# Value product of an attention stage: V made the stationary operand, exponentials streamed in two column tiles, results turned back by transposes

## Chip, cores, metric

The kernel runs on one core of one Trainium2 chip. The metric is the device time in microseconds of one execution. The profile is of one such execution and gives each engine's instructions: TensorE (PE, with its weight loads as PEld), VectorE (DVE), ScalarE (ACT), GpSimd (POOL) and SyncE (SP).

## The reference

Three stages follow one another. The change touches the first alone, masked attention over 2 x 8 = 16 heads with 768 tokens and head width 64, all in float32:

```python
mask = q_bucket[:, :, :, None] == k_bucket[:, :, None, :]      # 6 hash bits of q and k
scores = np.where(mask, scale * q @ k.T, -1e9)
scores = scores - np.max(scores, axis=-1, keepdims=True)
attn = np.exp(scores)
attn = attn / (np.sum(attn, axis=-1, keepdims=True) + 1e-09)
return np.matmul(attn, v)
```

A query that matches no key gets equal weights, that is the mean of V. The heads side by side form x (2 x 768 x 512). Then comes a Fourier transform over tokens and features, added to x, with a wide MLP behind it, and last a gated MLP that mixes tokens.

## The kernel before

**Tiling.** The 768 tokens of a head are T = 6 tiles of 128, or two halves of HALF = 384. For head g and key tile kt, `scores` makes transposed scores (keys on partitions, queries along the row) in two PSUM banks, one per half: four products of 384 columns in the type fp32r. ScalarE's `exponentials` writes exp of them to `E[:, kt % 3]`, 128 keys by 768 queries in float32. `values(t, ahead, kt)` multiplies: for each query tile j, the stationary operand is the 128 x 128 block `E[:, kt % 3, tile(j)]`, the moving one `vn[:, s, kt, :]` of D1 = 65 columns (64 of V and a column of ones, whose product is the row sum). The result, queries on partitions, accumulates over kt in one PSUM bank per head, alternating between two banks. A float32 product is issued as two instructions, each with its own weight load; an fp32r product is one instruction. So a head has 36 products, 72 instructions, of this kind. One product more, `ones` x `vsum`, gives the sum of V.

**Order.** Each engine has a program of its own, and semaphores join them. The heads are a software pipeline, `one_time(it, u)`: in one head time TensorE does the six `scores` of head g, the six `scores_for_max` of head g+2, the transposes and hash products of head g+3, `max_rows` of head g+1, and the value products of head g with one key tile of delay, so that the last (kt = 5) falls in the next head time. `first_times()` is the written-out start for the heads up to 0, a loop runs over heads 1 to 12, and four more head times (u = 1 to 4) finish heads 13, 14 and 15. Each engine works strictly through its own list.

**End of a head.** After the sixth value product, VectorE's `head_output` (L1283 to L1291) takes reciprocals of the row sums and scales the PSUM bank into X; this stands in its list at kt == 1. GpSimd's `finish_head` (L464, L467) then makes `fill`, the mean of V for queries with no match, and adds it to X, which raises `x_done`. GpSimd also sums V (L476 to L481), issues two copies of operand halves and lowers a tile of W1 (L508), in a fixed order.

**Last heads.** In the head times u = 2 and u = 3 behind the loop, VectorE's list has, behind `head_output`, the folds of the Fourier stage (`fold_tokens` L1347, `fold_features` L1360, `fold_mirrored` L1367 to L1370). ScalarE has `fold_hi` between the exponentials of kt = 4 and kt = 5, and it waits for those folds; GpSimd has `fold_lo` (L524) at the end of its list for that head time. TensorE's next head can't start its scores until the exponentials of kt = 5 have emptied the score banks. After u = 4 TensorE goes on with `first_transform(0)`.

Of the kernel before, what the change touches and what calls it, by code (L numbers as in the profile page):

```python
# [21 lines left out]
D1 = D + 1  # L22
# [28 lines left out]
SLOTS = 4  # L51

# [6 lines left out]
def mixer_kernel(nc, q, k, v, proj, w_ch1, w_ch2, w_in, g_ln, w_sg, b_sg, w_out,  # L59
                 t1_hi, t1_lo, t2_hi, t2_lo, out):  # L60
    with ExitStack() as ctx:
# [32 lines left out]
        def run(at, *items):  # L94
            placed = []
            for name, shape, dt in items:
# [10 lines left out]
                   ("vn", [P, SLOTS, T, D1], F32), ("E", [P, 3, S], F32), ("mz", [P, 2, T, 2], F32R),  # L107
# [5 lines left out]
                   ("low_rows", [P, 2, HALF], F32), ("bit_off", [P, 2], F32))  # L113
# [7 lines left out]
        A = layout("a", t1 + attn + t2 + [("W1H", W1H_AT, [P, FT, KT, P], F32R),  # L121
# [49 lines left out]
        st_rdy, exp_done, vsum_step, pv_step = sems("st_rdy exp_done vsum_step pv_step")  # L171

        norm, pv_out, fill_done, x_done = sems("norm pv_out fill_done x_done")
# [74 lines left out]
        PV_FREE = 3  # L248
        OUT_FREE = 2
# [4 lines left out]
        ST_BANK, PV_BANK, SM_BANK, PREP_BANK = 0, 2, 4, 6  # L254

# [10 lines left out]
        MEAN_AT = 400  # L266
# [164 lines left out]
        def _(pool):  # L431
# [5 lines left out]
            pool.memset(A["vn"][:, :, :, D:D1], 1.0)  # L437
# [19 lines left out]
            def finish_head(t):  # L457

                g, s = t.head(-1), t.slot(-1)
                pool.wait_ge(pv_out, g + 1 + OUT_FREE)  # L460
# [3 lines left out]
                pool.tensor_tensor(A["fill"][:, :, :], z, mean, ALU.mult).then_inc(fill_done, 1)  # L464
                pool.wait_ge(fill_done, g + 1)
                xh = head_out(t.it, t.u - 1)
                pool.tensor_tensor(xh, xh, A["fill"][:, :, :], ALU.add).then_inc(x_done, 1)  # L467

# [13 lines left out]

            def one_time(it, u):
                t = Time(it, u)
                if not t.looped and t.it < 0:
# [7 lines left out]
                else:  # L493
# [6 lines left out]
                    if t.has(1):  # L500
                        sum_values(t, 1)
                if t.has(-1):
                    finish_head(t)
                if t.has(0):

                    f = t.head(0)
                    pool.wait_ge(w1_hi, f + 1)
                    pool.tensor_tensor(M1["W1L"][:, f, :, :], A["W1R"][:, f, :, :], rd(A["W1H"][:, f, :, :]),  # L508
                                       ALU.subtract).then_inc(w1_lo, 1)
# [104 lines left out]
        def _(pe):  # L614
# [85 lines left out]
            def values(t, ahead, kt, tiles=range(T)):  # L700
                g, s, bank = t.head(ahead), t.slot(ahead), PV_BANK + t.slot(ahead, 2)
                if kt == 0 and 0 in tiles:
                    pe.wait_ge(v_in[s], 32 * t.turn(ahead) + 32)
                    pe.wait_ge(vsum_step, 3 * g + 3)
                    pe.wait_ge(pv_out, g - 1 + OUT_FREE)

                    mm(PS[:, bank, MEAN_AT:MEAN_AT + D], ones[:, :], A["vsum"][:, s, :], True, True)
                pe.wait_ge(exp_done, 2 * T * g + 2 * kt + 2 + EXP_FREE)
                for j in tiles:
                    last = mm(PS[:, bank, j * D1:(j + 1) * D1], A["E"][:, kt % 3, tile(j)], A["vn"][:, s, kt, :],  # L710
                              False, kt == T - 1, skip_group_check=True)
                if T - 1 in tiles:
                    last.then_inc(pv_step, 1)
# [6 lines left out]
            def first_times():  # L720
# [3 lines left out]

                a, b = range(TH), range(TH, T)
# [34 lines left out]
                values(fill0, 0, 0, a)  # L760
                scores_for_max(fill1, 3)
                values(fill0, 0, 0, b)
# [3 lines left out]
                values(fill0, 0, 1, a)  # L766
                both(hash_bits, fill1, 1)
                scores_for_max(fill1, 5)
                values(fill0, 0, 1, b)
# [842 lines left out]
```

## Time and profile before

| | us |
|---|---|
| median of 3 runs | 773.26 (770.96 to 773.28) |
| profiled execution, its time | 773.6 |
| its span, first to last instruction | 771.8 |
| TensorE matmul busy | 756.7 (98%) |
| TensorE weight load busy | 695.7 (90%) |
| VectorE, ScalarE, GpSimd busy | 404.3, 277.4, 201.9 |

About 1.8 us of the profiled time lie outside the span. A matmul's record starts when its columns begin to stream; its end is modelled and overlaps the next, so the pace of a run of matmuls is read from starts: (length of a row less length of its last record) divided by (count less one). A row of the timeline may merge several instructions (xN).

### The profile page before, as it was taken

How to read it: one execution, taken by the hardware profiler on the slowest of the kernel's cores; microseconds unless marked ns; L12 is line 12 of the kernel's file. 1: busy time of each engine (PE TensorE's matmuls, PEld its weight loads, DVE VectorE, ACT ScalarE, POOL GpSimd, SP SyncE). 2: the span in 40 equal slices, each digit the busy share in tenths (PEclk: the TensorE clock that was granted, in tenths of full speed). 3: DMA queues.
4: the chain of work that ended last, by engine and by line, in shares of the span. 5: the costliest groups of instructions: out<-in, count | busy, mean ns of one | idle time of the engine just before them, and what ended most of it. 6: DMA issues, size and time to landing. Idle time of an engine off the chain costs nothing.

```text
span 771.8 us, 12918 instructions
## 1 busy us (share of the span) xinstructions
PE 756.7 (98%) x4614; PEld 695.7 (90%) x4614; DVE 404.3 (52%) x746; ACT 277.4 (36%) x585; POOL 201.9 (26%) x258
## 2 busy tenths in 40 slices
PE   8999999999999999899999999999999999999998
PEld 7889999999999989899999999989999887888886
DVE  7887777677776658731132214123113487337733
ACT  4456666666665543411121112111113453015401
POOL 4133223332233563395000000000013146003300
PEclk9999999999999999999999999999999999999999
DMA  5233333223311500260000000000031000010001
GB/s 126 57 86 82 86 74 79 70 65 91 82 44 45 192 2 1 82 247 0 1 0 0 0 0 1 0 0 0 1 123 55 15 1 1 27 56 0 0 14 68
DMA packets 55569, 36.14 MB, mean 47 GB/s; under 512 B 40048, under 2 KB 48240, under 8 KB 55024
## 3 DMA queue, kind: packets, MB, share of 16 engines
q1 hardware_dynamic: 52720, 26.76, 12.2%
q0 software_dynamic: 2816, 8.94, 4.3%
q8 instruction: 21, 0.34, 0.2%
q14 instruction: 12, 0.10, 0.0%
HBM read 27.03 MB, written 3.15 MB: 39 GB/s over the span
## 4 chain that ended last, share of the span: by engine, by line
PE 90%; DVE 7%; issue 1%; ACT 1%; POOL 1%; DVEq 0%; POOLq 0%; ACTq 0%
PE PS L616 86%; DVE mneg L1264 2%; PE PS L631 1%; DVE ops L1244 1%; DVE Z L1360 1%; PE PS L937 1%; PE PS L979 1%; PE PS L883 1%; PE PS L905 1%; DVE fold L1347 0%; DVE Y L1367 0%; DVE ops L1234 0%; DVE Y L1368 0%; DVE ops L1231 0%; POOL vr L574 0%
## 5 line engine op out<-in xcount | busy, mean ns | idle before, releaser
L616 PEld LDWEIGHTS PS<-vn,E 128*128 128x128 f32 x1152 | 140.9, 192 | 1.6 <-ACT E L1037 1.4
L616 PE MATMUL PS<-vn,E 128*128 128x65 f32 x1152 | 140.6, 271 | 1.3 <-ACT E L1037 1.3
L1450 DVE SCALAR_TENSOR_TENSOR hL<-PS,hH 128x384 fp32r<-128x384 f32 x64 | 35.7, 558 | 201.5 <-ACT hH L1160 201.5
L616 PE MATMUL PS<-ops 98*128 98x384 f32 (+1 forms) x576 | 128.3, 354 | 2.0 <-DVE mneg L1264 1.5
L1264 DVE TENSOR_REDUCE mneg<-PS 128x1 f32<-128x768 f32 x96 | 91.8, 958 | 52.2 <-PE PS L616 51.0
L1160 ACT ACTIVATE hH<-PS 128x384 fp32r<-128x384 f32 x64 | 31.5, 492 | 227.2 <-PE PS L616 227.2
L1037 ACT ACTIVATE E<-PS 128x384 f32<-128x384 f32 x192 | 83.7, 487 | 77.5 <-PE PS L616 76.1
L616 PEld LDWEIGHTS PS<-ops 98*128 98x128 f32 (+1 forms) x576 | 96.5, 190 | 4.0 <-DVE mneg L1264 2.0
L616 PE MATMUL PS<-unTH,W1L 128*128 128x384 f32 x256 | 86.4, 337 | 0.0
L616 PE MATMUL PS<-unTH,W1H 128*128 128x384 f32 x256 | 86.2, 337 | 0.0
L616 PE MATMUL PS<-unTL,W1H 128*128 128x384 f32 x256 | 85.9, 336 | 0.0
L616 PE MATMUL PS<-W2H,hL 128*128 128x512 f32 x192 | 75.9, 395 | 0.0
L616 PE MATMUL PS<-W2L,hH 128*128 128x512 f32 x192 | 75.7, 395 | 0.0
L616 PE MATMUL PS<-W2H,hH 128*128 128x512 f32 x192 | 75.6, 394 | 0.0
L1023 ACT ACTIVATE ops<-PS 64x384 fp32r<-64x384 f32 (+1 forms) x96 | 44.8, 481 | 35.9 <-PE PS L616 20.8
L616 PEld LDWEIGHTS PS<-unTH,W1H 128*128 128x128 f32 x256 | 48.1, 188 | 2.6
L616 PEld LDWEIGHTS PS<-unTL,W1H 128*128 128x128 f32 x256 | 48.0, 188 | 2.5
L616 PEld LDWEIGHTS PS<-unTH,W1L 128*128 128x128 f32 x256 | 48.0, 188 | 0.0
L616 PEld LDWEIGHTS PS<-W2H,hL 128*128 128x128 f32 x192 | 36.0, 188 | 7.7
L616 PEld LDWEIGHTS PS<-W2L,hH 128*128 128x128 f32 x192 | 36.1, 188 | 6.0
L616 PEld LDWEIGHTS PS<-W2H,hH 128*128 128x128 f32 x192 | 36.1, 188 | 5.7
L565 POOL TENSOR_TENSOR WinL<-WinR,WinH 128x512 fp32r<-128x512 f32 x8 | 10.3, 1290 | 115.3 <-ACT WinH L1023 115.3
(178 smaller groups left out, 1298.7 us busy)
## 6 DMA issues: line engine op xcount, KB each, us to landing
ops<-ops POOLq DMA_DIRECT2D x28, 192.0 KB, 3.0
W1R<-in_moe_w_ch_dram SPq DMA_DIRECT2D x16, 256.0 KB, 2.8
W2R<-in_moe_w_ch_dram SPq DMA_DIRECT2D x4, 1024.0 KB, 6.9
qk<-in_k_dram SPq DMA_DIRECT2D x32, 96.0 KB, 2.8
qk<-in_q_dram SPq DMA_DIRECT2D x32, 96.0 KB, 2.8
vn<-in_v_dram SPq DMA_DIRECT2D x32, 96.0 KB, 2.8
out_dram<-X SPq DMA_DIRECT2D x12, 256.0 KB, 2.1
WsgR<-in_moe_w_sg_dram SPq DMA_DIRECT2D x1, 2304.0 KB, 7.9
```

The costliest lines, as they stand in the source:

```text
L565: pool.tensor_tensor(M2["WinL"][:, c // 2, cols], R1["WinR"][:, c // 2, cols], rd(M2["WinH"][:, c // 2, cols]), ALU.subtract).then_inc(win ...
L616: return pe.matmul(dst, lhs, rhs, start=start, stop=stop, **kw)
L631: last = pe.transpose(PS[:, bank, tile(c)], A["qk"][:, t.slot(3, 2), a * TH + c, :], ident[:, :])
L883: last = pe.transpose(PS[:, un_bank(n, kt), tile(c)], M1["un"][:, c, tile(kt)], ident[:, :])
L905: last = pe.transpose(PS[:, 5 + n % 3, tile(c)], R2["WsgR"][:, r, at:at + TH * (P - 1) + 1:TH], ident[:, :])
L937: last = pe.transpose(PS[:, 6 + j % 2, tile(kt)], M2["xs"][:, j % 2, tile(kt)], ident[:, :])
L979: last = pe.transpose(PS[:, 6 + j % 2, tile(kt)], M2["gated"][:, j % 2, tile(kt)], ident[:, :])
L1023: return act.activation(dst, src, ACT.Copy, scale=scale)
L1037: act.activation(A["E"][:, kt % 3, half(a)], PS[:, ST_BANK + a, 0:HALF], ACT.Exp, scale=EXP_SCALE).then_inc(exp_done, 1)
L1160: act.activation(M1["hH"][:, f % 2, :], PS[:, f % 2, 0:HALF], ACT.Relu).then_inc(hhi_done, 1)
L1264: dve.tensor_reduce(A["mneg"][:, s, j:j + 1], PS[:, max_banks(t, j):max_banks(t, j) + 2, 0:HALF], AX.XY, ALU.max, negate=True).then_inc(ma ...
L1450: dve.scalar_tensor_tensor(M1["hL"][:, f % 2, :], PS[:, f % 2, 0:HALF], 0.0, rd(M1["hH"][:, f % 2, :]), ALU.max, ALU.subtract).then_inc(hl ...
```

## The change

`values` now takes a part (0, 1, 2) of two key tiles each. V's tile (128 x 64) is stationary, and the exponentials stream past it, one half of 384 queries to the output partitions 0 to 63, the other to 64 to 127, in `PV_BANK`. The column of ones in `vn` goes. GpSimd adds exponentials over key tiles (`sum_exponentials`, four additions of 128 x 768 per head into `esumA` and `esumB`), and parts 1 and 2 multiply these with ones into `SUM_BANK`. `E` has four buffers in place of three. ScalarE copies both banks to `outT` (`raw_output`); TensorE turns them back (`turn_back`, at kt == 3 of the next head time): three transposes and three products of two columns for the row sums. VectorE's part is split into `value_mean` at kt == 1 and `head_output` at kt == 3. On GpSimd the fill and the lowering of W1 stand apart from `finish_head`, W1's one head later. The value parts of the first head and of each head time move to new places in TensorE's list.

```diff
+            def fill_head(t):
+                g, s = t.head(-1), t.slot(-1)
+                pool.wait_ge(mean_done, g + 1 + MEAN_FREE)
...
+            def sum_exponentials(t, ahead, step):
+                g = t.head(ahead)
+                dst = A["esumA"] if step < 2 else A["esumB"]
+                kt = (1, 2, 4, 5)[step]
+                pool.wait_ge(exp_done, 2 * T * g + 2 * kt + 2 + EXP_FREE)
+                if step % 2 == 0:
+                    if t.looped or g:
+                        pool.wait_ge(pv_step, PV_PARTS * (g - 1) + (2 if step == 0 else 3))
+                    first = A["E"][:, e_slot(t, ahead, kt - 1), :]
+                else:
+                    pool.wait_ge(esum_step, SUM_STEPS * g + step)
+                    first = dst[:, :]
+                pool.tensor_tensor(dst[:, :], first, A["E"][:, e_slot(t, ahead, kt), :], ALU.add).then_inc(esum_step, 1)
...
             def one_time(it, u):
                 t = Time(it, u)
+                if t.has(-1):
+                    sum_exponentials(t, -1, 3)
...
+                if t.has(0):
+                    sum_exponentials(t, 0, 0)
                 if t.has(-1):
+                    fill_head(t)
+                if t.has(0):
+                    sum_exponentials(t, 0, 1)
+                if t.has(-1):
+                    w1_lower(t)
                     finish_head(t)
                 if t.has(0):
...
+                    sum_exponentials(t, 0, 2)
...
+            def values(t, ahead, part):
+                g, s = t.head(ahead), t.slot(ahead)
+                if part == 0:
                     pe.wait_ge(v_in[s], 32 * t.turn(ahead) + 32)
+                    pe.wait_ge(mean_done, g + MEAN_FREE)
                     pe.wait_ge(vsum_step, 3 * g + 3)
+                    mm(PS[:, PV_BANK, MEAN_AT:MEAN_AT + D], ones[:, :], A["vsum"][:, s, :], True, True)
+                pe.wait_ge(exp_done, 2 * T * g + 4 * part + 4 + EXP_FREE)
+                for kt in (2 * part, 2 * part + 1):
+                    for a in range(2):
+                        last = mm(PS[a * D:(a + 1) * D, PV_BANK, 0:HALF], A["vn"][:, s, kt, :],
+                                  A["E"][:, e_slot(t, ahead, kt), half(a)], kt == 0, kt == T - 1)
+                if part:
+                    if part == 1:
+                        pe.wait_ge(pv_out, g + OUT_FREE)
+                    pe.wait_ge(esum_step, SUM_STEPS * g + 2 * part)
+                    sums = A["esumA"] if part == 1 else A["esumB"]
+                    for a in range(2):
+                        last = mm(PS[a * D:(a + 1) * D, SUM_BANK, 0:HALF], ones[:, 0:D], sums[:, half(a)],
+                                  part == 1, part == 2)
+                last.then_inc(pv_step, 1)
+
+            def turn_back(t):
+                g, s = t.head(-1), t.slot(-1)
+                pe.wait_ge(raw_done, g + 1)
+                for c in range(TH):
+                    pe.transpose(PS[:, SUM_BANK, tile(c)], A["outT"][:, 0, tile(c)], ident[:, :])
+                for c in range(TH):
+                    last = mm(PS[:, SUM_BANK, DEN_AT + 2 * c:DEN_AT + 2 * c + 2], A["outT"][:, 1, tile(c)],
+                              ident[:, 0:D + 1:D], True, True)
+                last.then_inc(ot_rdy, 1)
...
                 for kt in range(T):
                     if t.has(0):
                         scores(t, kt)
+                    if kt == 3 and t.has(-1):
+                        turn_back(t)
                     if t.has(2):
                         scores_for_max(t, kt)
...
-                    if kt == 0 and t.has(-1):
-                        values(t, -1, T - 1)
-                    if kt >= 1 and t.has(0):
-                        values(t, 0, kt - 1)
-                    if kt == 1 and t.has(1):
+                    if kt == 1 and t.has(-1):
+                        values(t, -1, 2)
+                    if kt == 2 and t.has(1):
                         max_rows(t, 0)
                         max_rows(t, 1)
+                    if kt in (3, 5) and t.has(0):
+                        values(t, 0, kt // 2 - 1)
...
+            def raw_output(t):
+                g = t.head(-1)
+                act.wait_ge(pv_step, PV_PARTS * g + PV_PARTS)
+                act.wait_ge(ot_rdy, g + TURN_FREE)
+                copy(A["outT"][:, :, :], PS[:, PV_BANK:PV_BANK + 2, 0:HALF]).then_inc(raw_done, 1)
...
                     if kt == 1 and t.has(-1):
-                        head_output(t)
+                        value_mean(t)
                     if kt in (3, 4) and t.has(3):
                         bit_rows(t, kt - 3)
+                    if kt == 3 and t.has(-1):
+                        head_output(t)
```

## Rows read from the trace of the kernel before

**Rows 1.** The page, busy shares and the granted clock in 40 slices.
```profile
PE 756.7 (98%) x4614; PEld 695.7 (90%) x4614; DVE 404.3 (52%) x746; ACT 277.4 (36%) x585; POOL 201.9 (26%) x258
...
PEclk9999999999999999999999999999999999999999
```

**Rows 2.** Stages: length, then busy us of PE, PEld, DVE, ACT, POOL; clock; DMA.
```profile
0.00:42.00 42.00, 37.33 (x248) 33.02 (x248) 33.56 (x62) 19.17 (x38) 12.55 (x31) 1.00 0.42 93
...
197.68:214.06 16.38, 16.38 (x127) 16.32 (x127) 12.41 (x26) 10.37 (x25) 5.38 (x9) 1.00 0.32 76
...
250.00:300.00 50.00, 47.69 (x363) 46.93 (x362) 30.03 (x46) 20.78 (x47) 28.17 (x22) 0.93 0.21 75
```

**Rows 3.** Groups by form on TensorE, 100 to 198 us: count, busy, mean ns.
```profile
L616 PE MATMUL PS<-vn,E 128*128 128x65 f32 x434 | 52.9, 271 | 0.0
```

**Rows 4.** Timeline of TensorE over one head time: start, length, count.
```profile
197.68 0.33 PE L616 MATMUL PS<-vsum,ones 128*128 128x64 f32 x2
197.85 1.50 PE L616 MATMUL PS<-vn,E 128*128 128x65 f32 x12
199.16 0.55 PE L616 MATMUL PS<-ident_r,mz 128*2 128x128 f32 x6
...
213.18 1.04 PE L616 MATMUL PS<-ops 128*128 128x384 f32 x5
214.06 0.33 PE L616 MATMUL PS<-vsum,ones 128*128 128x64 f32 x2
```

**Rows 5.** Timeline of TensorE in narrow windows, for the starts of successive float32 matmuls.
```profile
203.42 0.22 PE L616 MATMUL PS<-vn,E 128*128 128x65 f32 x1
...
203.47 0.39 PE L616 MATMUL PS<-vn,E 128*128 128x65 f32 x2
...
8.09 0.38 PE L616 MATMUL PS<-ident 128*128 128x128 f32 x2
...
8.20 0.50 PE L616 MATMUL PS<-ident 128*128 128x128 f32 x3
```

**Rows 6.** GpSimd: two groups by form, 50 to 250 us, then one of the timeline.
```profile
L467 POOL TENSOR_TENSOR X<-X,fill 128x384 f32 x12 | 12.0, 1002 | 3.8 <-POOL fill L464 3.8
L464 POOL TENSOR_TENSOR fill<-nomatch,vmean 128x384 f32<-128x384 f32 x13 | 10.8, 830 | 15.4 <-DVE X L1291 15.4
...
261.05 2.28 POOL L464 TENSOR_TENSOR fill<-nomatch,vmean 128x384 f32<-128x384 f32 x1 [3.76 <-DVE X L1291]
```

**Rows 7.** Timeline of the head time u = 2 (head 14), all engines.
```profile
257.51 0.95 PE L616 MATMUL PS<-ops 98*128 98x384 f32 x4
258.15 0.87 ACT L1037 ACTIVATE E<-PS 128x384 f32<-128x384 f32 x2 [1.52 <-PE PS L616]
259.79 0.17 DVE L1283 TENSOR_SCALAR den<-PS 128x6 f32<-128x6 f32 x1 [1.96 <-PE PS L616]
260.89 1.75 DVE L1347 TENSOR_TENSOR fold<-X 128x1536 f32<-128x1536 f32 x1
268.69 0.15 DVE L1370 COPY Y<-Z 128x3 f32<-128x3 f32 x1
268.88 1.48 ACT L1023 ACTIVATE yHL<-Y 128x1536 fp32r<-128x1536 f32 x1 [1.11 <-DVE Y L1370]
270.37 0.85 ACT L1037 ACTIVATE E<-PS 128x384 f32<-128x384 f32 x2
270.98 0.94 PE L616 MATMUL PS<-ops 98*128 98x384 f32 x4 [0.43 <-ACT E L1037]
```

**Rows 8.** Timeline behind head 15, and the stage 286 to 293 us.
```profile
284.17 3.43 POOL L524 TENSOR_TENSOR yHL<-Y,yHL 128x1536 fp32r<-128x1536 f32 x1 [3.46 <-ACT z0H L1023]
284.91 1.63 PE L616 MATMUL PS<-vn,E 128*128 128x65 f32 x12 [1.25 <-ACT E L1037]
286.30 0.51 PE L616 MATMUL PS<-T1H,yHL 128*128 128x194 f32 x1
...
286.00:293.00 7.00, 7.00 (x38) 6.77 (x37) 3.48 (x8) 0.59 (x2) 6.31 (x5) 0.52 0.00 0
```

**Rows 9.** The chain that ended last, 0 to 60 us, by line.
```profile
by line: PE PS L616 48.3%; DVE mneg L1264 20.9%; DVE ops L1244 10.6%; issue 4.9%; DVE ops L1234 4.7%; DVE ops L1231 4.0%; PE PS L631 3.3%; ACT ops L1023 0.8%; POOL ident L435 0.5%; DVE pjL L1297 0.4%; POOL ident L432 0.3%; POOL pj L433 0.2%
```

More of the change, by code:

```diff
@@ L21 @@
 FT = F // P
-D1 = D + 1
 LN_EPS = 1e-6
@@ L51 @@
 SLOTS = 4
+E_SLOTS = 4
 def token_tiles(ap):
@@ L247, in mixer_kernel @@
         EXP_FREE = 2
-        PV_FREE = 3
-        OUT_FREE = 2
+        MEAN_FREE = 1
+        TURN_FREE = 1
+        OUT_FREE = 1
         MAX_FREE = 1
@@ L254, in mixer_kernel, with e_slot @@
         ST_BANK, PV_BANK, SM_BANK, PREP_BANK = 0, 2, 4, 6
+        SUM_BANK = PV_BANK + 1
+        PV_PARTS, SUM_STEPS = 3, 4
+        def e_slot(t, ahead, kt):
+            return (T * t.slot(ahead, 2) + kt) % E_SLOTS
         def max_banks(t, j):
@@ L467, in finish_head, with w1_lower @@
                 pool.tensor_tensor(xh, xh, A["fill"][:, :, :], ALU.add).then_inc(x_done, 1)
+            def w1_lower(t):
+                f = t.head(-1)
+                pool.wait_ge(w1_hi, f + 1)
+                pool.tensor_tensor(M1["W1L"][:, f, :, :], A["W1R"][:, f, :, :], rd(A["W1H"][:, f, :, :]),
+                                   ALU.subtract).then_inc(w1_lo, 1)
             def sum_values(t, step):
@@ L704, in values @@
                     pe.wait_ge(vsum_step, 3 * g + 3)
[L705 to L711, printed above, removed]
@@ L1034, in exponentials @@
                     act.wait_ge(st_rdy, 2 * T * g + 2 * kt + a + 1)
-                    if a == 0:
-                        act.wait_ge(pv_step, T * g + kt - 2 + PV_FREE)
-                    act.activation(A["E"][:, kt % 3, half(a)], PS[:, ST_BANK + a, 0:HALF], ACT.Exp,
+                    if a == 0 and kt % 2 == 0 and (t.looped or g or kt == T - 2):
+                        act.wait_ge(pv_step, PV_PARTS * g + kt // 2 - 1)
+                    if a == 0 and kt in (1, T - 2) and (t.looped or g or kt == T - 2):
+                        act.wait_ge(esum_step, SUM_STEPS * (g - 1) + 3 if kt == 1 else SUM_STEPS * g + 1)
+                    act.activation(A["E"][:, e_slot(t, 0, kt), half(a)], PS[:, ST_BANK + a, 0:HALF], ACT.Exp,
                                    scale=EXP_SCALE).then_inc(exp_done, 1)
@@ L1057, in rows_of_maximum @@
                          PS[0:2, row_bank(t, a), 0:HALF]).then_inc(m_done, 1)
+            def raw_output(t):
+                g = t.head(-1)
+                act.wait_ge(pv_step, PV_PARTS * g + PV_PARTS)
+                act.wait_ge(ot_rdy, g + TURN_FREE)
+                copy(A["outT"][:, :, :], PS[:, PV_BANK:PV_BANK + 2, 0:HALF]).then_inc(raw_done, 1)
             def w1_upper(t):
@@ L1090, in one_time @@
                         upper_halves(t)
-                    if kt == 1 and t.has(1):
+                    if kt == 1 and t.has(-1):
+                        raw_output(t)
+                    if kt == 2 and t.has(1):
                         rows_of_maximum(t)
@@ L1277, in split_maximum, with value_mean @@
                                   ALU.subtract).then_inc(split_done, 1)
[L1279 to L1285 removed]
+            def value_mean(t):
+                g = t.head(-1)
+                dve.wait_ge(raw_done, g + 1)
+                dve.wait_ge(x_done, g - 1 + X_FREE)
+                dve.tensor_scalar(A["vmean"][:, t.slot(-1, 2), :], PS[:, PV_BANK, MEAN_AT:MEAN_AT + D], 1.0 / S, None,
+                                  ALU.mult).then_inc(mean_done, 1)
+            def head_output(t):
+                g, s = t.head(-1), t.slot(-1)
+                dve.wait_ge(ot_rdy, g + 1 + TURN_FREE)
+                den = PS[:, SUM_BANK, DEN_AT:DEN_AT + T].rearrange("p (c a) -> p a c", a=2)
+                dve.tensor_scalar(A["den"][:, :].rearrange("p (a c) -> p a c", a=2), den, DEN_EPS, None, ALU.add).then_inc(norm, 1)
                 dve.wait_ge(norm, 3 * g + 1)
```

55 lines of the change are left out of this document (18 added, 37 removed).

## The prediction

> **What bounds the kernel now.** First the page: TensorE has matmuls in flight for 98% of the span, at the full 2.4 GHz (granted clock 9 tenths or more in every slice) [rows 1]. Then the busy table by stage, to see whether that holds where the change acts. One steady head time, from one product of `vsum` to the next, takes 214.06 - 197.68 = 16.38 us [rows 4]. In it TensorE is never idle, VectorE is busy 12.4, ScalarE 10.4, GpSimd 5.4 us [rows 2]. So in the loop TensorE's own list sets the pace. In the start the chain of waits is shared with VectorE (20.9% in `mneg` alone) [rows 9], and in the last heads TensorE has pauses (47.69 busy in 50 us) and the clock's mean drops to 0.93 [rows 2]. These three stretches are costed apart. Then the timeline row by row.
>
> **What is removed.** Twelve value matmuls start at an even pace of (1.45 to 1.50 less 0.27) / 11 = 0.112 us [rows 3, 4]. The two shortest steps of the trace show why: behind 384 columns, whose time hides a weight load, the second matmul of 65 columns starts 0.05 to 0.06 us after the first [rows 5]; the steady 0.112 is the load of 128 float32 columns. So 72 x 0.112 = 8.05 us per head go.
>
> **What is added on TensorE.** No float32 matmul of 384 columns exists in the trace. Those of 65 columns take 0.055 us, those of 128 take 8.20 - 8.09 = 0.11 [rows 5], both 0.86 ns per column. The fp32r ones of 384 columns start every (1.04 - 0.34) / 4 = 0.175 us, 0.46 ns per column, with 0.015 above a plain 0.16 [rows 4]. A float32 stream thus costs two cycles a column, and 384 columns 0.32 + 0.015 = 0.335 us, call it one unit. Bounds: 0.175 if the doubling vanished, 0.34.
>
> A head has 6 x 2 value products and 2 x 2 sum products, 32 instructions. If nothing runs side by side that is 32 units, 10.7 us. If the two column tiles run fully side by side it is 16 units, 5.36 us. I take the tiles as independent but matmuls as starting in the order of the list. Then of each half its two instructions follow each other in the same tile, and only the second of one half overlaps the first of the other. A part of two key tiles takes 5 units, not 4; with its sums 7, not 6. Per head 5 + 7 + 7 = 19 units, 6.37 us. No row shows column tiles at work, which is the largest doubt here.
>
> By the Trainium skill (TensorE: Matmul & The Clock Gate, measured speedup of packing), three column tiles gave 2.38 times the rate; as an estimate two would give 1.59, so 32 / 1.59 = 20 units, 6.7 us. No row here shows it, and my sum doesn't use it.
>
> `turn_back` is three transposes and six matmuls, all with 128 stationary columns: 9 x 0.11 = 1.0 us. The mean's product stays.
>
> TensorE now changes between full width and half width six times a head. The nearest row is the group with two stationary columns: twelve value matmuls from 197.85 should end at 199.19 and the next group starts at 199.16 [rows 4], so a change of width there cost nothing that shows. The other bound is a full emptying of the array, about 271 - 112 = 159 ns, the part of a record that overlaps the next [rows 3]. I take 0.02 each, 0.1 a head, as the nearest row is near zero. The Trainium skill (TensorEngine Tiling (Array Packing), key properties) says a change of tiling mode drains the engine. By that the six would cost up to 1.0 us a head; it is a rival below.
>
> Steady head: -8.05 + 6.37 + 1.0 + 0.1 = -0.6 us. Thirteen head times run so (heads 1 to 13): -7.8 us.
>
> **What hides the rest.** Four additions of 128 x 768 per head on GpSimd: 384 elements take 1.00 us and 1536 take 3.43 [rows 6, 8], so 768 about 1.8, and 7.2 a head. GpSimd then has 12.6 of 15.8 us, and in order: it waits for operand halves until some 3.8 us into the head time (transposes to 1.7, then four ScalarE copies of 0.49), does its small work to 6.2, the first sum to 8.0, fill, second sum to 10.7, W1, finish to 13, third sum to 14.8, and the fourth ends 0.9 us into the next. TensorE asks for the last at 4.4 and for the second at 14.5, so both are hidden by over 3 us. Uncovered, each would put its whole 1.8 us on TensorE's path. ScalarE's copy of 768 columns, some 0.82 us (half of 0.87 plus a little, 0.49, for 384; 1.48 for 1536) [rows 7], brings it to 11.2. Its result is asked for two key tiles later. VectorE's work stays at 12.4. A load of V waits for the end of a head three back, which stays far in the past, so SP's queue is not moved.
>
> **The start.** Twelve units replace 60 matmuls (4.0 against 6.7 us), but much of this stretch follows VectorE's chain [rows 9], and the exponentials of kt = 4 now wait for GpSimd's first sum, which stands behind the operand copies; `max_rows` copies and hash bits queue behind them on ScalarE. I count +0.5 us, bounds -2 and +3.
>
> **The last heads: the cost.** In u = 2 `head_output` starts 259.79 - 257.51 = 2.3 us after the head time does. Behind it in VectorE's list are the folds, until 268.8; ScalarE's `fold_hi` waits for them, 268.88 to 270.4; behind it are the last exponentials, and behind these the next head's scores at 270.98 [rows 7]. So these head times (13.5 us) are set by this chain and not by TensorE, and what delays `head_output` delays everything. It now follows `turn_back`. Built up from the start: scores 0.7, scores of kt = 1 held by the exponentials to 1.65, part 2 to 4.0, ScalarE's copy to 4.9, exponentials (0.87 a pair) to 5.8, scores of kt = 3 to 6.15, `turn_back` to 7.15. That is 4.9 us later. In u = 3 the same 4.9, and more: GpSimd's fourth sum now stands behind `fold_lo`, 3.4 us long after `fold_hi`, so TensorE gets it at 5.0 and not 3.3, +1.7. After head 15, the value product took 286.30 - 284.91 = 1.4 us before the transform began [rows 8]. Now: `fold_lo` to 2.9 us, fourth sum to 4.7, its product 0.7, copy 0.9, turning 1.0, so 7.5, +6.1. Together 4.9 + 6.6 + 6.1 = 17.6. A pause of 1.25 us was followed by 7 us at clock 0.52, that is at 1.2 GHz [rows 8]; pauses of 4 to 5 us before u = 3 and in u = 4 put part 2 and the turning at half rate, about +2.4 beyond what was lost before. Tail: +20 us. Bounds: +14, if the clock holds and the sums find room; +27, if GpSimd's additions beside VectorE's folds stretch both (a fill there took 2.28 us in place of 0.83 [rows 6]).
>
> **Sum.** 773.6 - 7.8 + 0.5 + 20 = 786.3, against the profiled 773.6; the runs' median of 773.26 is 0.3 lower, so 786.
>
> **Rivals.**
> - *Each width change empties the array.* Six times 0.16 in place of 0.02, +0.85 a head, thirteen times: +11, 797. For it: the page named above. Against it: the row at 199.16.
> - *The tiles do not overlap.* 32 units: -8.05 + 10.7 + 1.1 = +3.8 a head, +49; the tail some 24, the start +3: about 850. For it: no row of column tiles. Against it: nothing in the rows but that weight loads of the next matmul run beside the present one.
> - *The tiles overlap without the stagger* (the other side). 16 units of 0.325, 5.2 us: -1.8 a head, -23, less the tail's 19: about 769, faster. It decides once a head saves more than 20 / 13 = 1.5 us. For it: the two tiles use separate banks of rows in PSUM. Against it: a float32 product's two instructions share a tile and start in order. A stream of one cycle a column would give about 743; rows 5 speak against it.
> - *The tail's loss just cancels the loop's gain*, for instance tail 14 and -1 a head: about 774.
>
> **How the numbers follow.** Chances: my forecast 0.50, emptying 0.14, no overlap 0.15, no stagger or a fast stream 0.15, cancelled 0.06. The forecast's own range is 776 to 798. The range 766 to 806 leaves out the case without overlap and 0.05 at the edges. A measurement of this kernel can tell 0.3%, 2.3 us, from no change: faster 0.15, same 0.06, slower 0.79.
>
> **What would show it.** Right: pairs of value matmuls with 0.33 us between two starts and two that start nearly together; a head time of 15.7 to 15.9 us with TensorE busy throughout; no TensorE wait for `esum` in the loop; in u = 2 and u = 3 head times of 18 us or more, with TensorE waiting for E while ScalarE waits for Y; a dip of the clock there; the first transform 7 us or more after the last exponentials. Wrong: starts evenly 0.33 apart, head times near 20 us; or head times below 15 us; or GpSimd's additions well over 2 us each, which would make GpSimd the bound at 2.5 us.

## The result, and the profile after

The changed kernel takes 839.57 us (median, 839.06 to 842.45) against 773.26: ratio 1.087, 95% interval 1.084 to 1.091. The forecast was 786 with a range of 766 to 806, so the time lies 34 us above the range. The profiled execution is the longest of four (842.45 us) and has a span of 840.6 us (771.8 before).

The page of the kernel after: busy time, the granted clock in 40 slices, the chain that ended last by engine, and one group of VectorE (busy us, mean ns, idle time ahead).

```profile
PE 777.5 (92%) x4118; PEld 626.1 (74%) x4118; DVE 443.5 (53%) x746; ACT 289.2 (34%) x601; POOL 317.5 (38%) x321
...
PEclk9989999999999898699999999999999999999999
...
PE 71%; DVE 11%; issue 10%; POOL 5%; ACT 1%; DVEq 1%; POOLq 0%; ACTq 0%
...
L1322 DVE TENSOR_SCALAR ops<-ops,bit_off 12x768 fp32r<-12x768 f32 x24 | 45.0, 1913 | 0.0
```

Three things differ from [rows 1]. TensorE is no longer busy nearly throughout (92% for 98%). VectorE's busy time rose by 39 us with the same 746 instructions, so some of them became longer. One group alone explains 31 of these: the subtraction of `bit_off`, 24 times 1.91 us; in the kernel before, the same 24 instructions took 0.60 each (shortest, median, longest in ns; from and to in us):

```profile
L1258 DVE TENSOR_SCALAR ops<-ops,bit_off x24: 600/604/607, 60.8 to 241.2; 12x768 fp32r<-12x768 f32 x24
```

What TensorE waited for, in the kernel after and, last row, in the kernel before (us in total, times, longest):

```profile
PE PS L659 <- DVE mneg L1328: 32.7, 28, 2.2
PE PS L659 <- ACT E L1092: 12.9, 6, 6.0
...
PE PS L659 <- POOL esumB L518: 1.8, 1, 1.8
...
PE PS L616 <- DVE mneg L1264: 1.5, 5, 0.5
```

The wait for `mneg`, the maximum, was 1.5 us in five waits before; it now comes about twice a head and makes 32.7 us. The second row is mainly the two long waits of the last heads. The busy table, one head time of the kernel after (from one product of `vsum` to the next; columns as in [rows 2]), and the end of the last head:

```profile
200.16:219.96 19.80, 17.62 (x97) 12.09 (x97) 15.16 (x26) 11.07 (x24) 13.02 (x13) 0.91 0.26 63
...
343.00:361.00 18.00, 11.51 (x46) 8.20 (x47) 3.14 (x11) 3.73 (x7) 11.17 (x7) 0.53 0.01 1
```

A head time that was 16.38 us [rows 2] is 19.80. TensorE has 2.2 us of idle time in it and a mean clock of 0.91. The timeline of the kernel after shows how that comes about (start, length; in brackets the idle time before it and what ended it):

```profile
210.05 0.62 PE L659 MATMUL PS<-ops 76*128 76x384 f32 x2 [2.07 <-DVE mneg L1328]
...
211.10 2.27 PE L659 MATMUL PS<-ops 98*128 98x384 f32 x6
...
215.95 1.33 PE L659 MATMUL PS<-ops 98*128 98x384 f32 x6
...
220.22 1.51 PE L659 MATMUL PS<-E,vn 128*64 128x384 f32 x8
...
224.81 1.82 POOL L518 TENSOR_TENSOR esumB<-E 128x768 f32<-128x768 f32 x1
...
225.28 3.86 DVE L1322 TENSOR_SCALAR ops<-ops,bit_off 12x768 fp32r<-12x768 f32 x2
...
226.71 2.02 POOL L518 TENSOR_TENSOR esumB<-esumB,E 128x768 f32<-128x768 f32 x1
226.97 0.98 PE L659 MATMUL PS<-ops 98*128 98x384 f32 x4
...
229.17 0.96 DVE L1328 TENSOR_REDUCE mneg<-PS 128x1 f32<-128x768 f32 x1
...
230.18 0.62 PE L659 MATMUL PS<-ops 76*128 76x384 f32 x2 [2.23 <-DVE mneg L1328]
```

Read it from GpSimd. Its third addition starts at 224.81. VectorE's first subtraction starts at 225.28, inside it, and ends only after it (at 227.04 by its own record, against 226.63). The second meets the fourth addition and ends at 229.14, after 228.73. So `mneg` of the next head, next in VectorE's list, starts at 229.17, and TensorE, which needs the bank that this maximum reads, stands idle for 2.23 us until 230.18. One head earlier it is the same (2.07 us until 210.05), and what follows shows there: the clock is granted at half rate, 1.2 GHz, and six products take 2.27 us at 211.10 that take 1.33 at full clock at 215.95. Such a half-rate stretch of 3.4 us stands in most head times.

By the first exponentials of each head (before, then after; us), the 68.8 us between the two spans fall like this:

| stretch | before | after | more | forecast |
|---|---|---|---|---|
| start, to head 1 | 46.5 | 53.1 | +6.6 | +0.5 |
| heads 1 to 13, 12 head times | 196.7 | 233.0 | +36.3 | -7.2 |
| u = 1 | 14.95 | 20.6 | +5.7 | -0.6 |
| u = 2, u = 3 and up to the transform | 28.2 | 49.0 | +20.8 | +20 |
| the rest | | | -0.6 | 0 |

The tail came as forecast. The loop has the wrong sign, and the start is outside its bounds.

### The profile page after: what moved, and what is told of

Same layout as the page of the kernel before. It is cut to its first block, busy times and chain, and to the rows that moved or that the text cites. A ratio compares the mean times of both kernels' runs of the same rounds, so it can differ in the third digit from the quotient of the medians.

```text
span 840.6 us, 12169 instructions
## 1 busy us (share of the span) xinstructions
PE 777.5 (92%) x4118; PEld 626.1 (74%) x4118; DVE 443.5 (53%) x746; ACT 289.2 (34%) x601; POOL 317.5 (38%) x321
## 4 chain that ended last, share of the span: by engine, by line
PE 71%; DVE 11%; issue 10%; POOL 5%; ACT 1%; DVEq 1%; POOLq 0%; ACTq 0%
PE PS L659 67%; DVE mneg L1328 3%; DVE ops L1322 3%; POOL esumB L518 2%; DVE ops L1315 2%; PE PS L674 1%; POOL esumA L518 1%; POOL X L482 1%; PE PS L990 1%; PE PS L1032 1%; PE PS L936 1%; PE PS L769 1%; PE PS L958 0%; DVE ops L1308 0%; DVE wgt L1358 0%
## 5 line engine op out<-in xcount | busy, mean ns | idle before, releaser
L659 PE MATMUL PS<-ops 98*128 98x384 f32 (+1 forms) x576 | 149.8, 386 | 40.3 <-DVE mneg L1328 32.7
L659 PEld LDWEIGHTS PS<-ops 98*128 98x128 f32 (+1 forms) x576 | 103.4, 206 | 82.7 <-DVE mneg L1328 41.2
L659 PE MATMUL PS<-E,vn 128*64 128x384 f32 x384 | 81.1, 548 | 6.0 <-ACT E L1092 6.0
L659 PEld LDWEIGHTS PS<-E,vn 128*64 128x64 f32 x384 | 25.7, 150 | 38.5 <-issue 27.4
L1322 DVE TENSOR_SCALAR ops<-ops,bit_off 12x768 fp32r<-12x768 f32 x24 | 45.0, 1913 | 0.0
```

The lines of the kernel that those rows point to most:

```text
L659: return pe.matmul(dst, lhs, rhs, start=start, stop=stop, **kw)
L1322: dve.tensor_scalar(rows, rd(rows), A["bit_off"][BITROW:KMAX, key:key + 1], None, ALU.subtract).then_inc(mask_done, 1)
```

## The experiments

The median of the kernel before beside these runs was 772.2 to 773.5 us. Kernels 1, 3, 4, 6 and 7 were executed once, the others 4 to 10 times. The theory throughout is that GpSimd's additions hold up VectorE's subtractions; against it stood the later place of `head_output`, a list of GpSimd that had become too long, and TensorE's own new work. "Head time" is the distance of two heads' first exponentials in the loop; the one from head 1 to head 2, which differs from the others, is left out. In 2, 3, 4, 8 and 9 the time came out 0.2 to 3.9 us above the range of the theory that held, in 5 and 7 it came out 0.1 and 7.4 us below.

**1. Short sums.** GpSimd's four additions per head cover 64 of 768 columns.

```diff
...
-                pool.tensor_tensor(dst[:, :], first, A["E"][:, e_slot(t, ahead, kt), :], ALU.add).then_inc(esum_step, 1)
+                pool.tensor_tensor(dst[:, 0:D], first, A["E"][:, e_slot(t, ahead, kt), 0:D], ALU.add).then_inc(esum_step, 1)
...
```

> The changed kernel, with GpSimd's four additions per head cut from 768 columns to 64 (the row sums are then wrong). Theory A: the loop is slow because GpSimd's long additions keep VectorE's SBUF-to-SBUF subtraction (L1322, 1.91 us instead of 0.60) from running, VectorE's chain reaches over the next head's first maximum, TensorE pauses and drops to 1.2 GHz. Then the subtraction is back at 0.60 us, a head time falls from 19.5 to 15.3-16.2 us, and the time to 775-790 us. Theory B: VectorE's chain is too long because head_output moved between the hash bits and the maxima of kt 3 and 4; then the head time stays above 18.5 us and the time above 820 us.

784.74 us. The head time falls to 15.9 to 16.1 (one of 16.4), the subtraction to 0.64 us, the time to head 1 from 53.1 to 48.9. The row sums are wrong in this kernel. Fifty-five of the 66 us hang on how long GpSimd's additions last. Which neighbour they hurt, this run doesn't tell.

**2. Sums behind the bits.** The full additions stay; the third only waits until VectorE has subtracted.

```diff
                 if t.has(0):
+                    if t.has(3) and (t.looped or t.it >= 0):
+                        pool.wait_ge(mask_done, 2 * t.head(3) + 2)
                     sum_exponentials(t, 0, 2)
```

> The changed kernel with one wait more: GpSimd starts the third addition of a head only when VectorE's subtraction of the hash rows is done; all work stays. Theory A (the two must not run together): subtraction 0.60 us, head time 15.5-16.5 us, 785-800 us in all. Theory B (position of head_output): no change, 835-845 us. Theory C (GpSimd's list is simply too long, 13 us a head): later additions make it worse, over 845 us.

800.24 us, ratio to before 1.036 (1.034 to 1.038). With the same work and one wait more, 39 us come back. The trace of this kernel, VectorE's subtraction by tile (ns: shortest, median, longest) and the timeline of the same place:

```profile
L1324 DVE TENSOR_SCALAR ops<-ops,bit_off x24: 600/604/606, 66.6 to 247.5; 12x768 fp32r<-12x768 f32 x24
```

```profile
198.03 1.13 DVE L1324 TENSOR_SCALAR ops<-ops,bit_off 12x768 fp32r<-12x768 f32 x2
199.19 0.96 DVE L1330 TENSOR_REDUCE mneg<-PS 128x1 f32<-128x768 f32 x1
199.41 1.83 POOL L518 TENSOR_TENSOR esumB<-E 128x768 f32<-128x768 f32 x1 [1.79 <-DVE ops L1324]
200.19 1.08 DVE L1336 CAST mz<-mneg 128x6 fp32r<-128x6 f32 x1
```

The maximum at 199.19 reads PSUM and takes its usual 0.96 us while the addition runs. The CAST of six columns at 200.19 has both operands in SBUF; it takes 1.08 us, not 0.17, and ends with the addition (201.27 against 201.24). So instructions of VectorE that work within SBUF can stand still during an instruction of GpSimd; those that read PSUM don't. Not all within SBUF do. In the kernel after, beside GpSimd's lowering of W1:

```profile
181.48 1.29 POOL L488 TENSOR_TENSOR W1L<-W1R,W1H  x1
...
182.00 0.19 DVE L1356 RECIPROCAL rec<-den 128x6 f32<-128x6 f32 x1
182.23 0.57 DVE L1358 TENSOR_TENSOR wgt<-rec,match 128x6 f32<-128x6 f32 x1
```

The reciprocal has both operands in SBUF and takes its usual 0.19 us; the product of two SBUF tiles behind it takes 0.57 for 0.17. Held in these traces are the subtraction, the CAST and instructions with two inputs in SBUF. In kernel 2 the head time is 16.3 to 16.8 and the clock no longer falls in the loop.

**3. The subtractions on ScalarE**, behind its last exponentials; the additions stay where the change put them.

```diff
...
+                    act.activation(rows, rd(rows), ACT.Identity,
+                                   bias=A["neg_off"][BITROW:KMAX, key:key + 1]).then_inc(mask_done, 1)
...
```

> The changed kernel with the two subtractions of L1322 moved from VectorE to the end of ScalarE's list for a head time; the additions stay where they were. Theory A: it is these two instructions that are kept from running, so the head time falls to 15.8-16.5 us though GpSimd is as busy as before, and the time to 788-800 us. If the additions disturb VectorE in another way too (reductions or products out of PSUM), the head time stays above 17.5 us and the time above 812 us.

800.55 us, head time 16.3 to 16.5 (one of 18.8). One head of this kernel:

```profile
214.41 1.83 POOL L518 TENSOR_TENSOR esumB<-E 128x768 f32<-128x768 f32 x1
214.70 1.75 ACT L1125 ACTIVATE ops<-ops,neg_off 12x768 fp32r<-12x768 f32 x2
216.31 1.88 POOL L518 TENSOR_TENSOR esumB<-esumB,E 128x768 f32<-128x768 f32 x1
```

ScalarE works within SBUF beside the same additions, at 0.9 us each and without being held. Two quite different edits that only part the subtractions from the additions give the same 800. Neither edit shortens GpSimd's list or moves `head_output`, so a list of GpSimd that had become too long, or the later place of `head_output`, is not what holds up the loop.

**4. Idle products in the pause.** Eight products of 112 columns into unused columns of `SUM_BANK`, ahead of the maximum's scores.

```diff
+                    if kt == 0 and t.has(2) and (t.looped or t.it >= 0):
+                        for _ in range(8):
+                            mm(PS[:, SUM_BANK, 400:512], ident[:, :], ident[:, 0:112], False, True, skip_group_check=True)
```

> The changed kernel with eight idle float32 products (16 matmuls of 112 columns, 1.8 us) on TensorE at the place of its pause, before the first scores for the maximum of each head. If the drops of the clock behind the pauses are a cost of their own, the stretches at 1.2 GHz vanish from the loop and the slow heads (19.9 us) come down to about 18.5: 820-828 us. If the clock is only a by-product, the time stays at 836-842 us.

831.23 us. The subtraction is still at 1.92 us. The half-rate stretches are gone from the loop and the head time is 18.6 to 18.9. So the clock is worth some 8 us of the loss, and the pause itself, with VectorE's chain behind it, the rest of what the loop lost.

**5. The same addition in the kernel before.** Three additions of 128 x 768 on data that nobody uses, behind the exponentials of kt = 4.

```diff
...
+                    pool.wait_ge(exp_done, 2 * T * g + 10 + EXP_FREE)
+                    for n in range(3):
+                        pool.tensor_tensor(A["dumB"][:, :], A["dumA"][:, :], A["dumA"][:, :], ALU.add).then_inc(dum, 1)
...
```

> The kernel before, with three idle GpSimd additions of 128x768 in a row behind the exponentials of kt 4 in each head time of the loop; nobody waits for them. Theory A: the subtraction (L1258 there, 0.60 us) grows to 1.2-2.2 us, VectorE's last maximum of a head comes 1-2 us later, head time 16.36 to 17-18 us, 782-795 us in all. Theory B: the subtraction stays at 0.60 us and the time at 772-775 us.

781.88 us, ratio 1.011 (1.010 to 1.013). Head time 17.17 for 16.36. By tile, and in the timeline:

```profile
L1270 DVE TENSOR_SCALAR ops<-ops,bit_off x24: 600/1208/1818, 60.4 to 249.9; 12x768 fp32r<-12x768 f32 x24
```

```profile
213.57 5.15 POOL L520 TENSOR_TENSOR dumB<-dumA 128x768 f32<-128x768 f32 x3
215.05 2.34 DVE L1270 TENSOR_SCALAR ops<-ops,bit_off 12x768 fp32r<-12x768 f32 x2
```

Nothing of the change but the additions is in this kernel, on other tensors, and the same instruction is held. It is the additions as such, not `E`, PSUM or the new order.

**6. Half by half.** On top of 2, the four instructions of one half before the four of the other.

```diff
-                for kt in (2 * part, 2 * part + 1):
-                    for a in range(2):
+                for a in range(2):
+                    for kt in (2 * part, 2 * part + 1):
```

> The kernel with the sums behind the hash bits (800 us), with the value products of a part in another order: both key tiles of the first half of the queries, then both of the second. If matmuls only run side by side with the next in the list, as the prediction had it, a part's eight matmuls take 7 x 0.32 us in place of 4, head time +2.9 us, and the time 835-845 us. If what runs side by side are the two matmuls of one float32 product, nothing changes: 797-803 us.

800.0 us: no change. In the after kernel value matmuls start in pairs 6 to 7 ns apart, 0.32 us from pair to pair. Here they start in pairs 13 ns apart, again 0.31 to 0.32 us from pair to pair, and a part still takes four steps. I first read this as the two instructions of one float32 product running side by side, whatever the tile. Run 7 tests that.

**7. One tile.** On top of 2, both halves go to partitions 0 to 63, in one accumulation; the upper 64 partitions of the output stay stale, and the attention output is the sum of two halves.

```diff
-                        last = mm(PS[a * D:(a + 1) * D, PV_BANK, 0:HALF], A["vn"][:, s, kt, :],
-                                  A["E"][:, e_slot(t, ahead, kt), half(a)], kt == 0, kt == T - 1)
+                        last = mm(PS[0:D, PV_BANK, 0:HALF], A["vn"][:, s, kt, :],
+                                  A["E"][:, e_slot(t, ahead, kt), half(a)], kt + a == 0, kt + a == T)
...
```

> Edit: the kernel in which GpSimd's third addition stands behind VectorE's bit subtractions (800.24 us, head time 16.4), and in it both halves of the value products and of the sums go to the output partitions 0 to 63; so the two halves are summed into one result, the upper 64 partitions of the output are stale, and attention is wrong for every query. The number and shape of the matmuls stay. Theory (the two instructions of one float32 product with 64 stationary columns run beside each other, whichever column tile they write): starts stay in pairs some 10 ns apart, 0.32 us from pair to pair, time 799 to 802. Rival (the overlap needs both column tiles, as the prediction assumed): the matmuls start evenly 0.32 apart, 32 units a head instead of 16, some 5 us more per head, 870 us or more.

862.61 us, and the rival's picture: even starts 0.32 us apart, 32 units a head, head time 20.9. Part 2 of this kernel, then of kernel 6:

```profile
203.87 2.79 PE L661 MATMUL PS<-E,vn 128*64 128x384 f32 x8
206.50 1.45 PE L661 MATMUL PS<-esumB,ones 128*64 128x384 f32 x4
```

```profile
201.59 1.52 PE L661 MATMUL PS<-E,vn 128*64 128x384 f32 x8
202.93 0.82 PE L661 MATMUL PS<-esumB,ones 128*64 128x384 f32 x4
```

So my reading of run 6 falls, and the column tiles do work side by side: exactly twofold here. Together the two runs say more. When the second tile's first matmul is two instructions behind in the list, it starts 6 to 7 ns after the first tile's; when it is four behind, 13 ns. That fits some 3.3 ns for each instruction passed, and a matmul that doesn't wait until those ahead of it in the list for the other tile have started. The records don't name the tile, so this order is inferred, not seen: from the two spacings, and from four steps for eight matmuls of which the list has four of one tile ahead of four of the other. The sums of kernel 6, whose order wasn't changed, start 13 ns apart as well, so the distance may simply be carried on from the products ahead of them.

**8. The tail.** On top of 2, VectorE folds tokens and features at the start of the head times u = 2 and u = 3 and mirrors behind `value_mean`; `fold_lo(1)` stands behind the last addition.

```diff
...
+                if not t.looped and tail_pass(t) is not None:
+                    n = tail_pass(t)
+                    dve.wait_ge(x_done, H + X_FREE)
+                    fold_tokens(n)
+                    fold_features(n)
                 for kt in range(T):
...
+                    if kt == 1 and not t.looped and tail_pass(t) is not None:
+                        fold_mirrored(tail_pass(t))
...
-                if not t.looped and tail_pass(t) is not None:
-                    fold_lo(tail_pass(t))
+                if not t.looped and tail_pass(t) == 0:
+                    fold_lo(0)
...
```

> The kernel with the sums behind the hash bits (800 us), with the last heads mended: in head times u = 2 and 3 VectorE folds before it waits for the turned-back outputs, and GpSimd's second fold_lo stands behind the last head's last addition. Theory: of the 27 us by which the stretch from head 14 to the first transform is longer than before (48.6 against 28.2 us from the first exponentials of head 14), most is head_output's new place ahead of the folds. Then u = 2 and u = 3 take 13-15 us each and the time is 783-789 us. If TensorE's or ScalarE's own work is the bound there, over 795 us.

790.12 us, ratio 1.021 (1.020 to 1.023): 10 us back. The edit moves two things. u = 2, where only the folds moved, takes 15.0 us in place of 19.6. From the last exponentials' end to the first transform, where `fold_lo` moved, it is 4.7 us in place of 9.0. u = 3 up to there is 1.5 us longer.

**9. And the start.** On top of 8, in the written-out start GpSimd makes the first two additions ahead of its wait for operand halves.

```diff
...
+                    if t.has(0):
+                        sum_exponentials(t, 0, 0)
+                        sum_exponentials(t, 0, 1)
                     if t.head(3) >= 2:
                         pool.wait_ge(hi_done, 4 * t.head(3) + 4)
                         move_halves(t)
...
```

> The last one, with the start mended too: for head 0 GpSimd makes its first two additions before it waits for the operand halves of head 3. The first exponentials of head 1 then come at 47-48 us in place of 51-53 us (before: 46.5), and the time is 779-786 us, still a little above the kernel before, because a head time of 16.4 us saves nothing on one of 16.36. If GpSimd was not what delayed the start: as the tail alone.

789.89 us, ratio 1.021 (1.020 to 1.023). Head 1 starts at 48.8 in place of 51.3. Not all of the 2.5 us are the edit's: kernel 8 runs 6.9 us at half clock before head 1, kernel 9 only 3.4. Kernel 6, whose GpSimd list for the start is the one of 8, also has 3.4 us at half clock there, and head 1 at 50.0. So at the same clock the queue position of that addition held the start by 1.2 us (one execution each); the whole time doesn't gain by it beyond what can be told. What is left stands in u = 3 of this kernel:

```profile
280.15 3.41 POOL L574 TENSOR_TENSOR yHL<-Y,yHL 128x1536 fp32r<-128x1536 f32 x1
...
283.68 1.79 POOL L518 TENSOR_TENSOR esumB<-esumB,E 128x768 f32<-128x768 f32 x1
283.80 4.98 DVE L1441 TENSOR_TENSOR Z<-fold 128x768 f32<-128x768 f32 x2 [6.26 <-POOL z0L L576]
285.44 2.53 POOL L518 TENSOR_TENSOR esumA<-E 128x768 f32<-128x768 f32 x1
...
285.53 1.55 PE L666 MATMUL PS<-esumB,ones 128*64 128x384 f32 x4 [5.16 <-POOL esumB L518]
```

`fold_lo` stands ahead of the fourth addition and TensorE waits 5.2 us for it. Beside VectorE's folds both sides stretch: the addition to 2.53 us for 1.8, and two folds of features to 4.98 us, where in kernel 11 below, with nothing beside them, two take 1.83.

**10. All mended, sums nearly free.** Kernel 9 with the short additions of 1 (row sums wrong for most queries).

> Edit: all mended orders together (third addition behind the bit subtractions, first head's additions before the operand copies, folds first in the last heads; 789.89 us so far), and GpSimd's additions cut to 64 of 768 columns; the other 704 columns of the sums hold constants, so the row sums are wrong for most queries. It shows what the rest of the change is worth when the additions cost nothing. Theory (what keeps a head time at 16.3 us is still the additions beside VectorE's work, and the additions behind fold_lo in the tail): head time 15.1 to 15.9, tail 4 us shorter, 770 to 778 us: no better than before, as the turning back and the longer chain at the tail eat TensorE's gain. Rival (the order of the list, not the additions, holds the head time at 16.3): head time 16.2 or more, 785 or more.

771.42 us, ratio 0.999 (0.998 to 1.001). One head time of this kernel:

```profile
185.80:201.70 15.90, 15.61 (x96) 10.93 (x95) 12.39 (x26) 10.91 (x24) 6.52 (x12) 1.00 0.32 78
```

VectorE is back at 12.4 us and TensorE's own list is 15.6, 0.8 below the 16.38 of [rows 2]. That is what the new value product is worth at best. Both kernels reach the first transform at 286.3 us: the start takes 1.1 us more, the twelve head times 3.2 less (16.1 each on average, with waits, for 16.4), and the stretch from there 2.2 more, of which 1.9 lie behind head 15's first exponentials (16.6 us to the transform for 14.7).

**11. The kernel before with folds first.** The VectorE part of 8 in the kernel before, with the mirrors behind `head_output`.

> Edit: the kernel before, with the folds of tokens and features at the head of VectorE's list in the head times u = 2 and u = 3 and the mirrored fold behind head_output. It tells whether the tail of the kernel before also follows the chain head_output, folds, fold_hi, exponentials. Theory: ScalarE's fold_hi waits 1.1 us less, the next scores start 1 to 3 us earlier in each of the two head times: 768 to 771 us. Rival (GpSimd's fold_lo or TensorE's own list sets the tail; VectorE's folds meet GpSimd's work and head_output comes later): 773 or more.

768.63 us, ratio 0.995 (0.994 to 0.997): the one version that beats both kernels. Its trace:

```profile
257.76 1.75 DVE L1348 TENSOR_TENSOR fold<-X 128x1536 f32<-128x1536 f32 x1
...
259.54 1.83 DVE L1361 TENSOR_TENSOR Z<-fold 128x768 f32<-128x768 f32 x2
...
267.67 1.49 ACT L1023 ACTIVATE yHL<-Y 128x1536 fp32r<-128x1536 f32 x1
...
284.20 0.34 PE L616 MATMUL PS<-T1H,yHL 128*128 128x194 f32 x1
```

ScalarE's `fold_hi` starts at 267.67, not at 268.88, and no longer waits; the transform begins at 284.20 and not at 286.30, and the half-rate stretch behind it [rows 8] is gone from there; one of half its length (3.4 us for 6.8) comes at 296.

## Why the prediction was wrong

**The step that failed: "VectorE's work stays at 12.4"** (What hides the rest). In a head time it is 15.2 us. GpSimd's additions of 1.8 us were sized rightly and "hidden" in GpSimd's own list and for TensorE, also rightly: no wait for `esum` stands in the loop. But they were not hidden from VectorE. They were priced as if each engine had SBUF to itself, and the last two stand beside VectorE's subtractions, the last work ahead of the next head's first maximum. Each is held by 1.3 us, 2.6 a head; TensorE then pauses 2.1 us, and the half clock costs more. Experiments 2, 3 and 5 show it from three sides. The warning was in the rows: a `fill` beside VectorE's folds took 2.28 us in place of 0.83 [rows 6]. I used it as a bound of the tail alone. The Trainium skill (SBUF — State Buffer, SBUF: two separate sides) has VectorE and GpSimd share a port pair that is locked for a whole instruction, on VectorE's side only by instructions in a two-port mode or with two inputs in SBUF, while ScalarE has ports of its own. The traces agree, with 0.60 us become 1.6 to 2.2 beside an addition, the reciprocal's 0.19 us unchanged and ScalarE's 0.9 us unheld. The prediction cited other pages of the Trainium skill and not this one, which was the one that bore on the change.

**Size of the loop's loss.** From 16.36 to some 19.7 us a head: the waits for `mneg` are 11.3 us in the five head times from 109.5 to 208 us, 2.3 each. With TensorE's own 15.6 that makes 17.9. Four of these five head times have a half-rate stretch of 3.4 us and take 19.8 to 20.0 us, the one without takes 18.7, so a stretch costs 1.25 us, 1.0 a head on average; some 0.8 a head stays unaccounted. Removing the half clock gave 8 us in all (experiment 4), parting additions and subtractions 39 with the clock (experiment 2). Heads 1 to 13 and u = 1 together lost 42.

**TensorE's own sum: -0.6 forecast, -0.8 found, and three of its four terms off.**
- Removed: 8.05 forecast. By starts, [rows 4] has the twelve from 197.85 to 199.16 at 1.31, and the other five groups take 1.26 each, so 7.6. Counting 72 full steps of 0.112 was too much: in five of the six groups the first step is 0.06 us [rows 5], and the step from each group's last to the next row is 0.08.
- Added: 19 units forecast, 16 found. "Matmuls as starting in the order of the list" is refuted by 6 and 7. A unit is 0.322, not 0.335, so 5.15 for 6.37. The Trainium skill (TensorEngine Tiling (Array Packing), key properties) says that tiles operate independently, and run 7 against run 2 agrees. The estimate of 20 units that the prediction made from the Trainium skill (TensorE: Matmul & The Clock Gate, measured speedup) was too dear.
- Width changes: 0.02 each forecast. In kernel 10 a start after a change comes 0.10 us later than without (0.27 for 0.17 into a value group, 0.42 for 0.32 out of one), and the first step within a group is 0.05 longer (0.37 for 0.32): three ways in with 0.15, three out with 0.10, 0.75 a head for 0.1. The row at 199.16 [rows 4] changed the stationary columns from 128 to 2 and was the wrong neighbour; the rival's 0.16 each was nearer.
- `turn_back`: 1.0 forecast, 0.92 found.
So -7.6 + 5.15 + 0.75 + 0.92 = -0.8, beside the 15.61 of the window. That the sum comes out near the forecast's -0.6 is luck: too high a gain, too high a cost and too low a price of the changes cancelled.

**The rivals.** "Tiles do not overlap" is refuted for the kernel after, and experiment 7 shows what it would cost: 62 us more than kernel 2, where the forecast had 850 - 786 = 64. "Width changes empty the array" was right in size and wrong in outcome, because "no stagger" was right as well; neither gives the sign of the loop. None of the four rivals had VectorE as the victim.

**The start: +0.5 forecast, +6.6 found.** The prediction had named the cause (exponentials of kt = 4 behind GpSimd's first sum, and the rows of the maximum behind these) and bounded it too low. In the kernel after, GpSimd reaches its first addition only at 41.10, behind the operand copies:

```profile
41.10 1.83 POOL L518 TENSOR_TENSOR esumA<-E 128x768 f32<-128x768 f32 x1
...
43.05 0.87 ACT L1092 ACTIVATE E<-PS 128x384 f32<-128x384 f32 x2 [3.31 <-POOL esumA L518]
```

TensorE then waits 1.5 us for `ops` and runs 6.8 us at half clock, and 3.4 us more at half clock lie from 30.2 to 33.6; the kernel before has no half rate between 6.3 us and head 1. The wait and half of these 10.2 us make the 6.6. How much half rate there is varies where the start's list is the same: 10.2 us in the kernel after, 6.8 in 2 and 3.4 in 6, with head 1 at 53.1, 51.3 and 50.0; why is not shown. The prediction had no term for the clock in the start. Putting the additions ahead of the copies gave 1.2 us at the same clock (experiment 9).

**The tail: +20 forecast, +20.8 found.** The chain is the one described: the value bank's result goes to `outT`, is turned back, then `head_output`, folds, `fold_hi`, exponentials, next scores. Timeline of the kernel after, u = 2:

```profile
314.68 2.32 DVE L1420 TENSOR_TENSOR fold<-X 128x1536 f32<-128x1536 f32 x1
...
317.04 4.12 DVE L1433 TENSOR_TENSOR Z<-fold 128x768 f32<-128x768 f32 x2
...
323.14 1.48 ACT L1076 ACTIVATE yHL<-Y 128x1536 fp32r<-128x1536 f32 x1 [6.45 <-DVE Y L1443]
...
325.24 3.20 PE L659 MATMUL PS<-ops 98*128 98x384 f32 x8 [5.79 <-ACT E L1092]
```

`head_output` starts 7.5 us after the head time does, where 7.15 was built up, and the first transform comes 9.0 us after the last exponentials' end (346.7 to 355.70) where 7.5 was. SBUF work is held here too: a fold of 1.75 takes 2.32, two of 1.83 take 4.12. But it was held before as well, beside `fill`, and from the first fold to the last copy it is 8.3 us for 7.8 [rows 7], so this is not what made the tail longer. By parts: u = 2 took 6.1 us more for a forecast of 4.9, u = 3 up to the last exponentials 7.2 for 6.6, and from there to the transform 7.6 for 6.1; the half clock, 2.4 in the forecast, is inside these. The 1.7 us of waiting for the fourth sum in u = 3 did not come (TensorE has one wait for `esumB`, 1.8 us, behind head 15), so the total is closer than its terms. Experiment 8 confirms the mechanism by taking 10 us back.

**What stays open.** In kernels 2 and 9 a head time is 16.3, 0.7 above TensorE's list; short waits for `mneg` are there (2.5 us between 109.5 and 208 us of kernel 2, six head times), and with short additions (kernel 10) they are 0.6 in the same stretch; that accounts for part of the 0.7 only. Over all twelve head times the mean is 16.5 in kernel 2 and 16.1 in kernel 10, so the full additions still cost 0.4 a head there, and 0.5 above TensorE's list remain even with short ones. Whether another place for the third and fourth addition would free the rest was not tried, nor were sums of `E` on TensorE in place of GpSimd's.

## What to carry to other kernels

Work put on GpSimd isn't free because GpSimd has time: list what VectorE does within SBUF at that moment, above all subtractions, casts and instructions with two SBUF inputs, and what waits for it. If a long addition of GpSimd must run, place it beside VectorE's reads of PSUM and let it wait for the short SBUF instructions ahead. Price a removed group of matmuls from its first start to the next group's, and check that the row you take for a change of width really changes the width of the tile.

## What the hardware showed unexpectedly

- A VectorE instruction of six columns within SBUF (0.17 us alone) took 1.08 us beside a 1.83 us addition of GpSimd, and one of 12 x 768 went from 0.60 to 1.6 to 2.2; reductions from PSUM kept their 0.96 us, and a reciprocal within SBUF its 0.19.
- Two column tiles of 64 gave exactly twice the rate for float32 products of 384 columns: 16 steps of 0.32 us for 32 instructions, in either order of the list. Each change between full and half width cost 0.10 to 0.15 us.
- A float32 stream takes 0.322 us for 384 columns, 0.84 ns a column at full clock.
